# Scaling the queries by 2^-20 in their split, and two VectorE passes with no statistic between them

## What is computed

```python
# q, k, v: (4, 8, 576, 64); tau: scalar; 32 heads in 16 pairs
scores = scale * np.matmul(q, k.transpose(0, 1, 3, 2))
thresh = np.max(scores, axis=-1, keepdims=True) - tau
scores = np.where(scores >= thresh, scores, -1000000000.0)
scores = scores - np.max(scores, axis=-1, keepdims=True)
attn = np.exp(scores)
attn = attn / (np.sum(attn, axis=-1, keepdims=True) + 1e-09)
x = np.matmul(attn, v)                       # then (2304 tokens, 512)
h = x @ w_in;  x = (h - np.tanh(h)) @ w_out        # 512 -> 2048 -> 512
h = x @ w_in2; x = (h / (1 + np.exp(-h))) @ w_out2 # 512 -> 2048 -> 512
```

## Time and profile before

| what | value |
|---|---|
| median of 3 runs | 1100.23 us (1100.09 to 1100.81) |
| the profiled execution, its own time | 1100.23 us |
| its span, first to last instruction | 1098.4 us |
| PE busy | 1076.1 us, 98% of the span |
| DVE busy | 559.1 us, 51% |
| ACT busy | 402.8 us, 37% |
| POOL busy | 265.5 us, 24% |
| granted TensorE clock | 1.000 over the span |

### The profile page before, as it was taken

One profiled execution on the slowest core, in us unless ns is written; L12 is line 12 of the kernel. 1 busy time (PEld: TensorE's weight loads), 2 busy tenths in 40 slices (PEclk: granted clock), 3 DMA queues, 4 the chain that ended last, 5 costly groups with the idle time before them and its releaser, 6 DMA issues.

```text
span 1098.4 us, 15693 instructions
## 1 busy us (share of the span) xinstructions
PE 1076.1 (98%) x5808; PEld 870.5 (79%) x5808; DVE 559.1 (51%) x1342; ACT 402.8 (37%) x830; POOL 265.5 (24%) x240
## 2 busy tenths in 40 slices
PE   5999999999999999999999999999999999999998
PEld 4667677676678888888888889888888888888898
DVE  7999999999767543343343344622322322222222
ACT  5889898888732211121121121422211211111111
POOL 3767676776254200000000000444000000000000
PEclk9999999999999999999999999999999999999999
DMA  6334242431142100000000000232100000010010
GB/s 153 81 74 111 57 111 66 102 89 36 58 147 96 58 1 1 1 0 0 0 0 0 0 1 1 89 111 70 39 1 1 28 10 0 0 38 0 0 39 20
DMA packets 15195, 46.38 MB, mean 42 GB/s; under 512 B 2080, under 2 KB 2592, under 8 KB 15136
## 3 DMA queue, kind: packets, MB, share of 16 engines
q1 hardware_dynamic: 15136, 45.62, 14.8%
HBM read 40.89 MB, written 4.72 MB: 42 GB/s over the span
## 4 chain that ended last, share of the span: by engine, by line
PE 95%; DVE 1%; ACT 1%; POOL 0%; issue 0%; DVEq 0%; ACTq 0%
PE hid L761 36%; PE acc L777 35%; PE scores L718 9%; PE pv L683 8%; PE tps L740 6%; DVE x_lo L605 0%; ACT w_parts L450 0%; ACT x_hi L459 0%; DVE probs L584 0%; DVE probs L552 0%; ACT pT L407 0%; POOL q_parts L361 0%; DVE w_parts L635 0%; DVE stats L568 0%; ACT pR L409 0%
## 5 line engine op out<-in xcount | busy, mean ns | idle before, releaser
L761 PE MATMUL hid<-x_hi,w_parts 128*128 128x512 f32 (+1 forms) x1280 | 384.9, 368 | 3.2 <-DVE x_lo L605 2.1
L777 PE MATMUL acc<-g_hi,w_parts 128*128 128x512 f32 (+1 forms) x1280 | 384.1, 368 | 0.0
L761 PEld LDWEIGHTS hid<-x_hi,w_parts 128*128 128x128 f32 x1280 | 234.2, 189 | 44.6 <-DVE x_lo L605 2.2
L777 PEld LDWEIGHTS acc<-g_hi,w_parts 128*128 128x128 f32 x1280 | 234.1, 189 | 39.9
L761 PE MATMUL hid<-x_lo,w_parts 128*128 128x512 f32 (+1 forms) x640 | 235.4, 368 | 0.0
L777 PE MATMUL acc<-g_lo,w_parts 128*128 128x512 f32 (+1 forms) x640 | 235.4, 368 | 0.0
L619 DVE CAST g_hi<-h_act 128x512 fp32r<-128x512 f32 (+1 forms) x160 | 71.2, 445 | 270.0 <-ACT h_act L474 267.3
L374 POOL TENSOR_TENSOR w_parts<-w_raw,w_parts 128x1024 fp32r<-128x1024 f32 x30 | 73.6, 2457 | 400.0 <-ACT w_parts L450 399.9
L614 DVE TENSOR_TENSOR h_act<-hid,h_act 128x512 f32<-128x512 f32 (+1 forms) x80 | 51.0, 638 | 200.8 <-ACT h_act L471 200.8
L471 ACT ACTIVATE h_act<-hid 128x512 f32<-128x512 f32 (+1 forms) x80 | 44.4, 555 | 293.3 <-PE hid L761 293.3
L474 ACT ACTIVATE h_act<-hid 128x512 f32<-128x512 f32 (+1 forms) x80 | 44.4, 555 | 290.0 <-PE hid L761 290.0
(11 more groups left out here) (46 smaller groups left out, 765.9 us busy)
## 6 DMA issues: line engine op xcount, KB each, us to landing
w_raw<-w_in SPq DMA_DIRECT2D x32, 512.0 KB, 3.4
k_raw<-k_in SPq DMA_DIRECT2D x30, 288.0 KB, 4.8
q_raw<-q_in SPq DMA_DIRECT2D x30, 288.0 KB, 5.9
v_all<-v_in SPq DMA_DIRECT2D x16, 320.0 KB, 3.1
out<-xT SPq DMA_DIRECT2D x4, 1024.0 KB, 4.2
k_raw<-k_in SPq DMA_DIRECT2D x4, 144.0 KB, 3.0
q_raw<-q_in SPq DMA_DIRECT2D x4, 144.0 KB, 2.9
out<-xT SPq DMA_DIRECT2D x1, 512.0 KB, 2.9
```

The costliest lines, as they stand in the source:

```text
L761: last = pe.matmul(hid[f % HBANKS][:, 0:w], a, b[:, kc, 0:w], start=(kc == 0 and i == 0), stop=(kc == KC - 1 and i == 2))
L777: last = pe.matmul(acc[n][:, 0:w], a, b[f % GRING][:, 0:w], start=(f == 0 and i == 0), stop=(f == FT - 1 and i == 2))
```

## The change

Queries are multiplied by 2^-20 when they are split, so the scores come out of PE already scaled. ACT does its part inside the copy (an immediate scale). The subtraction needs the same scale on `q_raw`; POOL therefore gets a pass of its own over the queries, in place, ahead of the normalisation of the same step, and for the first pair DVE's subtraction becomes one instruction that multiplies and subtracts. The first pass now subtracts `margin` (tau in the scaled unit), and what it accumulates with the maximum is the threshold itself. The second pass reads that threshold directly. The bias of the exponential is made of the threshold by a one-element instruction behind the second pass, and ACT's exponential waits for that too. The reciprocal now stands behind the second pass. `stats`, `stat_scale` and `stat_bias` are gone; the masked entries rest on 2^40 in place of 3e38 and on tau bounded by 110.

```diff
@@ POOL steps
+                    if what == "queries":
+                        pool.wait_ge(q_hi_done, 2 * g + h + 1)
+                        rows = q_raw[u][:, h]
+                        pool.tensor_scalar(rows, rows, FINE, 1.0, ALU.mult, ALU.mult).then_inc(q_fine, 1)
+
                     q = k - L_NORM
                     if here(q):
...
                     if what == "queries":
-                        pool.wait_ge(q_hi_done, 2 * g + h + 1)
+                        pool.wait_ge(q_fine, 2 * (g - 1) + h + 1)
@@ ACT steps
                         act.wait_ge(lift_done, n + 1)
-                        act.activation(tile, tile, ACT.Exp, bias=stats[:, c, 0:1], scale=-SCALE / FINE,
+                        act.wait_ge(bias_done, n + 1)
+                        act.activation(tile, tile, ACT.Exp, bias=exp_bias[:, c:c + 1], scale=-SCALE / FINE,
...
-                        act.activation(q_parts[u][:, h, 0:SEQ], q_raw[u][:, h], ACT.Copy).then_inc(q_hi_done, 1)
+                        act.activation(q_parts[u][:, h, 0:SEQ], q_raw[u][:, h], ACT.Copy, scale=FINE).then_inc(q_hi_done, 1)
@@ DVE prelude
-            dve.tensor_scalar(fine[:], tau_ok[:], FINE, None, ALU.mult)
-            for scale in stat_scale:
-                dve.memset(scale[:, 0:1], -SCALE / FINE)
-                dve.memset(scale[:, 1:2], 1.0 / FINE)
...
+            dve.tensor_scalar(tau_low[:], tau_ok[:], -UNMASKED, UNMASKED, ALU.mult, ALU.add)
+            dve.tensor_scalar(tau_high[:], tau[:], DEEPEST, FINE / SCALE, ALU.min, ALU.mult).then_inc(tau_steps, 1)
             dve.wait_ge(tau_steps, 2)
-            dve.tensor_tensor(stat_bias[:, 1:2], margin[:], tau_low[:], ALU.add).then_inc(tau_steps, 1)
+            dve.tensor_tensor(margin[:], tau_high[:], tau_low[:], ALU.max).then_inc(tau_steps, 1)
@@ DVE steps
-                        dve.tensor_scalar(tile, scores[q % SBUFS][:, :, 0:HALF], fine[:], None, ALU.mult, ALU.max,
-                                          accum_out=finemax[:, c:c + 1]).then_inc(max_done, 1)
+                        dve.tensor_scalar(tile, scores[q % SBUFS][:, :, 0:HALF], margin[:], None, ALU.subtract,
+                                          ALU.max, accum_out=thr[:, c:c + 1]).then_inc(thr_done, 1)
...
-                        dve.wait_ge(max_done, n + 1)
-                        dve.scalar_tensor_tensor(out=stats[:, c], in0=stat_scale[q % SBUFS], scalar=finemax[:, c:c + 1],
-                                                 in1=stat_bias[:], op0=ALU.mult,
-                                                 op1=ALU.add).then_inc(stats_done, 1)
+                        tile = probs[:, slot_of(q), :].rearrange("p (a s) -> p a s", a=2)
+                        dve.wait_ge(thr_done, n + 1)
+                        dve.scalar_tensor_tensor(out=tile, in0=scores[q % SBUFS][:, :, 0:HALF],
+                                                 scalar=thr[:, c:c + 1], in1=tile, op0=ALU.is_lt,
+                                                 op1=ALU.subtract).then_inc(lift_done, 1)
+                        dve.tensor_scalar(exp_bias[:, c:c + 1], thr[:, c:c + 1], -SCALE / FINE, None,
+                                          ALU.mult).then_inc(bias_done, 1)
...
-                        dve.wait_ge(stats_done, n + 1)
-                        dve.scalar_tensor_tensor(out=tile, in0=scores[q % SBUFS][:, :, 0:HALF],
-                                                 scalar=stats[:, c, 1:2], in1=tile, op0=ALU.is_lt,
-                                                 op1=ALU.subtract).then_inc(lift_done, 1)
@@ DVE, first pair
-                dve.tensor_tensor(rows, q_raw[0][DH:P, h], rows.bitcast(F32), ALU.subtract).then_inc(qk_split, 1)
+                dve.scalar_tensor_tensor(out=rows, in0=q_raw[0][DH:P, h], scalar=FINE, in1=rows.bitcast(F32),
+                                         op0=ALU.mult, op1=ALU.subtract).then_inc(qk_split, 1)
```

More of the change, by code:

```diff
@@ L18 @@
 SCALE = 1.0 / float(np.sqrt(DH))
-UNMASKED = 3.0e38
+UNMASKED = 2.0 ** 40
+DEEPEST = 110.0
 FINE = 2.0 ** -20
@@ L211, in build @@
         acc = [ctx.enter_context(nc.psum_tensor(f"acc{u}", [P, CHUNK], F32)) for u in range(KC)]
-        stat_scale = [tile[:, 1, HALF:HALF + 2] for tile in scores]
         def v_of(u, c, h):
@@ L231, in build @@
         scores_done = sem("scores_done")
-        max_done = sem("max_done")
-        stats_done = sem("stats_done")
+        q_fine = sem("q_fine")
+        thr_done = sem("thr_done")
+        bias_done = sem("bias_done")
         exp_done = sem("exp_done")
@@ L336, in steps @@
                 for k in ks:
+                    what, h = split_in(k - 1, first)
+                    g, u = PAIRS * B + k // TILES, k // TILES % 2
+                    if what == "queries":
+                        pool.wait_ge(q_hi_done, 2 * g + h + 1)
+                        rows = q_raw[u][:, h]
+                        pool.tensor_scalar(rows, rows, FINE, 1.0, ALU.mult, ALU.mult).then_inc(q_fine, 1)
                     q = k - L_NORM
@@ L346, in steps @@
                         pool.tensor_scalar(tile, tile, r, 1.0, ALU.mult, ALU.mult).then_inc(norm_done, 1)
-                    what, h = split_in(k - 1, first)
-                    g, u = PAIRS * B + k // TILES, k // TILES % 2
                     if what == "keys":
@@ L438, in _ @@
                 act.activation(k_hi[0][:, h], k_raw[0][:, h], ACT.Copy).then_inc(k_hi_done, 1)
-                act.activation(q_parts[0][:, h, 0:SEQ], q_raw[0][:, h], ACT.Copy).then_inc(q_hi_done, 1)
+                act.activation(q_parts[0][:, h, 0:SEQ], q_raw[0][:, h], ACT.Copy, scale=FINE).then_inc(q_hi_done, 1)
             steps(0, range(STEPS), True)
@@ L522, in _ @@
             dve.wait_ge(tau_steps, 1)
-            dve.tensor_scalar(fine[:], tau_ok[:], FINE, None, ALU.mult)
-            for scale in stat_scale:
-                dve.memset(scale[:, 0:1], -SCALE / FINE)
-                dve.memset(scale[:, 1:2], 1.0 / FINE)
-            dve.memset(stat_bias[:, 0:1], 0.0)
-            dve.tensor_scalar(tau_low[:], tau_ok[:], UNMASKED, -UNMASKED, ALU.mult, ALU.add)
-            dve.tensor_scalar(margin[:], tau[:], -1.0 / SCALE, tau_ok[:], ALU.mult, ALU.mult).then_inc(tau_steps, 1)
+            dve.tensor_scalar(tau_low[:], tau_ok[:], -UNMASKED, UNMASKED, ALU.mult, ALU.add)
+            dve.tensor_scalar(tau_high[:], tau[:], DEEPEST, FINE / SCALE, ALU.min, ALU.mult).then_inc(tau_steps, 1)
             dve.wait_ge(tau_steps, 2)
-            dve.tensor_tensor(stat_bias[:, 1:2], margin[:], tau_low[:], ALU.add).then_inc(tau_steps, 1)
+            dve.tensor_tensor(margin[:], tau_high[:], tau_low[:], ALU.max).then_inc(tau_steps, 1)
             dve.wait_ge(tau_steps, 3)
@@ L577, in steps @@
                         dve.reciprocal(rinv[:, cols], rowsum_e[:, cols]).then_inc(rinv_done, 1)
-                    q = k - L_S
-                    if here(q):
-                        n, c = STEPS * B + q, q % RING
-                        dve.wait_ge(stats_done, n + 1)
-                        tile = probs[:, slot_of(q), :].rearrange("p (a s) -> p a s", a=2)
-                        dve.scalar_tensor_tensor(out=tile, in0=scores[q % SBUFS][:, :, 0:HALF],
-                                                 scalar=stats[:, c, 1:2], in1=tile, op0=ALU.is_lt,
-                                                 op1=ALU.subtract).then_inc(lift_done, 1)
             for h in range(2):
```

7 lines of the change are left out of this document (3 added, 4 removed).

## The result

The changed kernel takes 1109.06 us (median of 4 executions, 1108.87 to 1109.13), against 1100.52 us for the kernel before in the same comparison (4 executions, 1100.09 to 1101.92). The ratio is 1.0074, 95% interval 1.0062 to 1.0086: **0.74% slower**. The forecast was 1108.2 us. The profiled execution took 1109.13 us and its span is 8.9 us longer than before.

What follows compares the result with a forecast made beforehand. PE's own work was taken to pace steady attention: 1100.23 us + 2.0 (start) + 6.0 (13 stalls of 0.46) = 1108.2 us. The forecast's own range was 1103.8 to 1112.3, widened to 1101 to 1113 for 8 in 10.

Steps and rivals of the forecast that it cites:

- What bounds the kernel: Steady attention: PE's own work sets the pace, with 0.28 us of slack behind DVE's second pass; time saved on DVE is idle.
- DVE's step: Attention on DVE: second pass at +0.86 us, period 1.73 in place of 1.84, 1.66 without reciprocal; worth nothing at the bound.
- Edits at nothing: ACT's copy scale, margin subtraction, exponential's second wait, shorter prelude and first pair's fused subtraction: all taken as 0 us.
- The sign that I named: In the profile after, ACT's exponential would not wait for the bias, written by +1.74 us.
- The stall of a pair: Steady pair: POOL's path behind ACT's copy grows 1.60 us, so PE's transposes wait 0.46 us for the next normalisation.
- The count: The stall comes with the query split for each of pairs 3 to 15: 13 times 0.46 = 6.0 us.
- The start: First pairs, where POOL runs through without waits: its new instructions delay scores and transposes, costing 2.0 us.
- Rival 1: Steady pairs: the normalisation still comes in time, no stall, only the start's cost; say 1101.6 us; chance 0.12.
- the slack of 1.19 us: Kernel before, steady pair: time from the end of tile j = 2's POOL normalisation to PE's transposes loading that tile.
- Rival 2: Steady attention: DVE paces PE after all, 0.25 us gained in each of 42 waits, faster at 1091.7 us; chance 0.07.
- Rival 3: POOL's new instruction runs like a two-input one, 1.42 us; stall 1.14, start 4.0, 1119 us in all; chance 0.06.
- Rival 4: DVE's period does not fall, bias and reciprocal at 0.13 us each; 1108.7 us, inside the forecast; no chance given.

Runs made afterwards that it cites:

- e2_no_pass: Changed kernel without POOL's pass over the queries, all of DVE's side kept (scores not the reference's): 1099.88 us, ratio 0.9991 to the kernel before.
- e6_dve_split: Changed kernel with the query rest made by DVE in one multiply-and-subtract instruction, POOL keeping only the first of the second pair: 1102.86 us, ratio 1.0016.
- e5_pe_busy: Changed kernel with 30 transposes of the identity added on PE, directly ahead of its wait before step 9: 1108.35 us, ratio 1.0068.
- e1_behind_norm: Changed kernel with POOL's pass over the queries moved behind the normalisation of its step, the work unchanged: 1104.22 us, ratio 1.0025.
- e7_by_one: Changed kernel with POOL's pass multiplying by 1.0 in place of 2^-20 (output not the reference's): 1108.09 us, ratio 1.0069.
- e10_mixed: Changed kernel with POOL's pass behind the normalisation, by 2^-10 twice, and DVE making two query parts near the start: 1099.68 us, ratio 0.9994.
- e3: Kernel before with only POOL's pass over the queries added, multiplying by 1.0, DVE's order untouched: 1108.57 us, ratio 1.0065.
- e4: Changed kernel with a second POOL pass over the queries, by 1.0, behind the first: 1122.27 us, ratio 1.0193.
- e9: Changed kernel with POOL's pass multiplying by 2^-10 twice in its one instruction, the same result as 2^-20: 1109.03 us, ratio 1.0079.

## Why the prediction held, point by point

**What bounds the kernel.** Right. PE paces steady attention: e2_no_pass takes 0.8 us of DVE's work out of a pair and the pair stays at 17.56 us. That there was slack is shown from the other side too: e6_dve_split puts 0.76 us into one step of DVE, and PE waits for only 0.08 us of it. The 0.28 us that I read from the earlier trace rows were not measured by themselves.

**DVE's step.** Right in its order and close in its size. One step of after in the start:

```profile
11.00 0.82 DVE L552 TENSOR_SCALAR_CACHE_REDUCE probs<-scores,margin 128x576 f32<-128x576 f32 x1
...
11.86 0.82 DVE L569 SCALAR_TENSOR_TENSOR probs<-scores,thr,probs 128x576 f32<-128x576 f32 x1
...
12.60 0.14 DVE L572 TENSOR_SCALAR exp_bias<-thr 128x1 f32<-128x1 f32 x1
12.66 0.81 DVE L552 TENSOR_SCALAR_CACHE_REDUCE probs<-scores,margin 128x576 f32<-128x576 f32 x1
```

The second pass stands at +0.86 as forecast, and the period without a reciprocal is 1.66. With it the period is 1.71, where I had 1.73: the two small instructions cost 0.06 and 0.05 us rather than 0.07 each.

**Edits at nothing.** Right in cost. The sign that I named, the exponential not waiting for the bias, did not come true as written: it is held by the new bias four times, in the first steps, 4.7 us in all; the kernel before had it held there by the second pass four times, 5.3 us. ACT's query copy with its scale takes 0.68 us as before, and behind the last scores nothing moved.

**The stall of a pair.** Right: forecast 0.46, measured 0.46 in the row above and 0.45 by the pair. The path is the one I had followed, but that the number fits to 0.01 us is in part luck, since two of its terms were off and cancel. POOL's path grew by 1.65 us where I had 1.60: 0.76 + 0.89, not 0.72 + 0.73 + 0.15. And the room behind ACT's copy was larger: before, the transposes loaded 4.42 us after the copy's start (210.71 to 215.13); in after they would have been due at 4.48 (217.79 to 222.73, less the wait of 0.46). The pass was costed by its likeness to the normalisation. It lasts less (0.67), and with this constant the next instruction starts later behind it (0.76).

**The count.** Thirteen stalls in the steady part, as summed. They come in the step that I named: the step from the scores of j = 7 is 2.74 us in place of 2.28. The second pair has two more, 0.45 and 0.81 us, which belong to the start.

**The start.** Right in mechanism, mis-sized: 3.0 us, forecast 2.0. The term that was too small is the distance from step 9 to the normalisations that follow, which I took from before with its clock. So the sum was 1.0 us short at the start and 0.1 us long on the stalls (5.9 against 6.0), 0.9 us in all. The places that I had named, forecast against after and e5_pe_busy:

| place | forecast | after | e5_pe_busy |
|---|---|---|---|
| scores of step 9 | 28.59 | 28.68 | 28.94 |
| normalisation of tile 8, behind step 9 | 4.59 | 5.20 | 4.56 |
| normalisation of tile 11, behind step 9 | 12.15 | 13.15 | 12.26 |
| transposes of tile 11, behind step 9 | 12.95 | 13.95 | 13.05 |

With PE kept busy every distance is within 0.11 us of the forecast. In after they are 0.6 to 1.0 us longer. The last two rows of after:

```profile
38.47 0.67 POOL L342 TENSOR_SCALAR q_raw<-q_raw 128x576 f32<-128x576 f32 x1 [0.35 <-ACT q_parts L439]
...
41.83 0.74 POOL L352 TENSOR_SCALAR probs<-probs,rinv 128x576 f32<-128x576 f32 x1 [0.30 <-POOL q_parts L365]
...
42.63 0.42 PEld L736 LDWEIGHTS tps<-ident,probs 128*128 128x128 f32 x4 [0.81 <-POOL probs L352]
```

The first late link is the scores of step 9 (complete 0.52 us later than with e5_pe_busy, counted from their start). ACT falls behind with them, and its copy then makes POOL wait 0.35 us, a wait that e5_pe_busy has not. I knew that PE's idle time would grow, from 1.12 us by at least 1.6, and did not ask what PE would do right behind it. The clock's share is shown by e5_pe_busy and the table beside it; that ACT's late copy follows from it is argued from the order of the rows. (The lower end of the range, with its own terms of 0.2 and 1.2 us, is 1104.0 and not 1103.8; nothing hangs on it.)

**The rivals.** Rival 1 (no stall) is false for the change, and e1_behind_norm is its mechanism made true: with only the pass ahead, the slack of 1.19 us is enough. Rival 2 (DVE paces PE) falls with e2_no_pass. The Trainium skill (Perfetto Trace Analysis, section Identifying the Most-Contended Engine) would judge PE by weight-load busy time, together with the share of its peak arithmetic that it delivers, rather than by matmul busy time. By the weight loads alone, as I used it, this points the wrong way in this kernel: they were 70% of the stretch and DVE 95%, yet shortening DVE moved nothing. Rival 3 (1.42 us for the pass) is false: 0.67. The estimate of 0.86 us from the figure of the Trainium skill's GPSIMD Engine Reference, section 3.1, is too high as well. Rival 4 is false, since the period fell, and as foreseen it would not have mattered.

## What to carry to other kernels

Before work is added to an engine that is half idle, follow its queue around the place: what matters is which instruction now stands behind it, how much slack the consumer of that one has, and whether the added instruction brings a wait to a place where the queue had run free. The same 0.67 us of POOL cost 0.45 us a steady pair ahead of a normalisation and nothing behind it; at the start, where POOL had no slack, it cost in either place. And when an edit makes PE idle longer, cost the products behind the gap at the lower clock too.

## What the runs showed of the hardware

**The clock behind a gap.** After 3.9 us of idle PE the granted clock was 0.72 over 26 to 32 us, the stretch with the first products behind the gap; with the gap filled it was 1.00. It was 0.72 too in e2_no_pass, where PE idled for 2.40 us, and 1.00 in before, behind 1.12 us. These are mixtures of the two levels, 1.2 and 2.4 GHz. The fall need not come at once: behind 3.58 us of idle PE, the first score product of step 9 took 0.40 us in e7_by_one, as at the full clock, and that of step 10 took 0.59. What it cost in after is the 0.89 us by which the stretch of e5_pe_busy from step 9 to 17 is shorter.

**The same gap, with and without a fallen clock.** The kernel before had executions at 1100.1 and at 1101.8, e10_mixed at 1099.5 and 1101.1. The profiles show a place where such a difference arises: at the start of the second network, behind a wait of PE for DVE of 1.74 us. First before, one of the shorter executions, then e5_pe_busy, its longest:

```profile
700.42:704.00 3.58, 3.58 (x16) 2.98 (x17) 1.94 (x5) 3.10 (x4) 1.99 (x1) 1.00 0.47 146
```

```profile
708.65:712.30 3.65, 3.65 (x9) 2.88 (x10) 1.82 (x4) 2.34 (x2) 2.35 (x1) 0.55 0.47 148
```

PE did 16 matmuls in one and 9 in the other, at clocks of 1.00 and 0.55, and the same 33 matmuls took 7.76 and 9.41 us, 1.65 apart. All twelve profiles have this wait, of 1.74 or 1.75 us; over the 3.6 us behind it the clock was 0.53 to 0.58 in five (e3, e4, e5, e9, e10) and 1.00 in the other seven. What decides it, these runs don't show, nor whether it is all of the scatter: e2_no_pass and e3_pass_alone have executions in between. For a comparison of 1 us, a place in the trace ahead of it is a better measure than a median.

**POOL.** A pass over 128x576 of fp32 takes 0.67 us with two immediates and 0.75 with a multiplier per partition. A normalisation behind a pass by 2^-20 starts 0.76 or 0.77 us after it, behind passes by 1.0, 0.5 or 2^-10 twice 0.64 to 0.66. And in e6_dve_split the normalisation beside DVE's query instruction, with two inputs in SBUF, took 1.20 us in place of 0.75, 26 times; the 19 normalisations of after between 20 and 60 us, beside DVE's passes with PSUM as an input, all lie between 0.742 and 0.755 us. That the DVE instruction is what lengthens it rests on their standing side by side.
